# Batch 0's sequence transform as cosine and sine sums, its butterfly in pieces, two more hidden transforms moved ahead of the MLP, powers loaded from ScalarE's queue

## What is computed

```python
# 1. attention with a decaying state, per block of positions
intra = (q @ k.T * D) @ v;  inter = (q * lam_pow) @ kv_state
kv_state = lam_block * kv_state + (k * rev_pow).T @ v
# 2. mixing by a Fourier transform, then an MLP
u = x + real(fft(fft(x, axis=1), axis=2))
un = (u - mean(u)) / sqrt(var(u) + 1e-6)
x = u + relu(un @ w_ch1) @ w_ch2            # 512 -> 2048 -> 512
# 3. a gated unit
gate = sigmoid(causal convolution of x with 5 taps)
out = (gate * (x @ w_val)) @ w_out
```

## Time and profile before

| what | value |
|---|---|
| median of 3 runs | 458.44 us (457.67 to 460.20) |
| the profiled execution's own time | 459.72 us |
| its span, first to last instruction | 457.9 us |
| mean granted TensorE clock | 0.988 |
| TensorE busy | 438.7 us, 96% |
| VectorE busy | 268.2 us, 59% |
| ScalarE busy | 151.9 us, 33% |
| GpSimd busy | 147.0 us, 32% |

### The profile page before, as it was taken

How to read it: one execution, slowest core, us unless ns; L and a number is a source line. 1 busy time by engine, 2 the same in 40 slices (tenths; PEclk the granted TensorE clock), 3 DMA queues, 4 the chain that set the end, 5 groups by cost and what they waited for, 6 DMA issues and landing times.

```text
span 457.9 us, 7070 instructions
## 1 busy us (share of the span) xinstructions
PE 438.7 (96%) x2892; PEld 420.1 (92%) x2892; DVE 268.2 (59%) x419; ACT 151.9 (33%) x284; POOL 147.0 (32%) x99
## 2 busy tenths in 40 slices
PE   6799859999999999999999999999999999999997
PEld 5688749989999999999999999999999999889985
DVE  1657993566835974643533424966565557999220
ACT  1154343065322141111524217344125134525312
POOL 1432536235523222332376422332422450600000
PEclk9899979999999999999999999999999999999999
DMA  6977810050220220202022022022022020001112
GB/s 209 320 219 269 289 67 2 1 183 20 73 94 0 93 77 16 92 1 94 1 93 92 1 92 94 0 93 92 1 92 93 0 93 2 0 1 70 69 47 92
DMA packets 14032, 37.05 MB, mean 81 GB/s; under 512 B 1576, under 2 KB 3120, under 8 KB 14000
## 3 DMA queue, kind: packets, MB, share of 16 engines
q1 hardware_dynamic: 14000, 36.60, 23.8%
HBM read 33.44 MB, written 3.15 MB: 80 GB/s over the span
## 4 chain that ended last, share of the span: by engine, by line
PE 87%; DVE 7%; DMA 3%; ACT 1%; issue 1%; SPq 1%; DVEq 0%
PE ps L550 10%; PE ps L552 9%; PE ps L573 9%; PE ps L572 9%; PE ps L571 9%; PE ps L551 9%; PE ps L489 3%; PE ps L657 2%; PE ps L656 2%; PE ps L655 2%; PE ps L433 2%; PE ps L408 2%; PE ps L634 2%; PE ps L635 2%; PE ps L636 2%; PE ps L444 2%
## 5 line engine op out<-in xcount | busy, mean ns | idle before, releaser
L741 ACT ACTIVATE hh<-ps 128x384 fp32r<-128x384 f32 x64 | 31.5, 492 | 173.1 <-PE ps L552 173.1
L1017 DVE SCALAR_TENSOR_TENSOR hl<-ps,hh 128x384 fp32r<-128x384 f32 x64 | 35.3, 556 | 83.3 <-ACT hh L741 83.3
L550 PE MATMUL ps<-cen_h,w1h_a 128*128 128x384 f32 x128 | 44.1, 344 | 0.5 <-DVE hl L1017 0.5
L550 PE MATMUL ps<-cen_h,w1h_b 128*128 128x384 f32 x128 | 44.2, 345 | 0.0
L552 PE MATMUL ps<-cen_h,w1l_b 128*128 128x384 f32 x128 | 43.1, 337 | 0.0
L552 PE MATMUL ps<-cen_h,w1l_a 128*128 128x384 f32 x128 | 43.1, 337 | 0.0
L573 PE MATMUL ps<-hh,w2l_b 128*128 128x384 f32 x128 | 43.1, 337 | 0.0
L572 PE MATMUL ps<-hl,w2h_b 128*128 128x384 f32 x128 | 43.1, 337 | 0.0
L571 PE MATMUL ps<-hh,w2h_b 128*128 128x384 f32 x128 | 43.1, 337 | 0.0
L551 PE MATMUL ps<-cen_l,w1h_a 128*128 128x384 f32 x128 | 43.1, 337 | 0.0
L551 PE MATMUL ps<-cen_l,w1h_b 128*128 128x384 f32 x128 | 43.0, 336 | 0.0
(11 more groups left out here) (179 smaller groups left out, 1045.5 us busy)
## 6 DMA issues: line engine op xcount, KB each, us to landing
raw_a<-in_mlp SPq DMA_DIRECT2D x16, 512.0 KB, 4.8
raw_b<-in_mlp SPq DMA_DIRECT2D x16, 512.0 KB, 4.4
chunks<-in_qkv SPq DMA_DIRECT2D x12, 512.0 KB, 5.5
chunks<-in_qkv SPq DMA_DIRECT2D x22, 256.0 KB, 4.9
out<-out_sb SPq DMA_DIRECT2D x12, 256.0 KB, 2.0
raw_a<-in_val SPq DMA_DIRECT2D x2, 512.0 KB, 4.5
raw_b<-in_out SPq DMA_DIRECT2D x2, 512.0 KB, 4.6
seq_c<-const_seq SPq DMA_DIRECT2D x1, 768.0 KB, 5.8
```

The lines of the kernel that those rows point to most:

```text
L550: mm(bank, wh_, xh, start=r == 0, stop=False)
L741: nc.scalar.activation(hh[:, slot, j], ps[j][:, 0:TB], ACT.Relu).then_inc(s_hh, 1)
L1017: stt(hl[:, slot, j], ps[j][:, 0:TB], 0.0, hh[:, slot, j].bitcast(F32), ALU.max, ALU.subtract).then_inc(s_hl, 1)
```

## The change

Batch 0 now uses `seq_pair` and `add_pair` too; `seq_tile`, `add_u` and the table part `seq_up` (512 KB) go. The butterfly's operations are the same, but stand at other places: two of the four of `two_pairs` at n = 6, the other two and pair 2 at n = 7, the last six at n = 8. Hidden transforms 6 and 7 move from behind `mean(0)` into chunks 9 and 10, 8 and 9 move behind `mean(0)`, 10 and 11 stay in the MLP; their `radix4` and `spectrum_copy` move along. Tile 2 and 3 of the sequence transform stand behind `from_chunk(10)`. The five instructions on the powers (a write, and three loads behind a wait for it) go from SyncE to the head of ScalarE's queue.

```diff
-            sp.wait_ge(s_pow, 2 + 7)
-            sp.dma_start(rv_dram, rv).then_inc(s_rv, 16)
             load(1, 0, 2, s_tin)
-            sp.wait_ge(s_rv, 16)
-            sp.dma_start(decay[:, :, :], ...
-            for par in range(2):
-                sp.dma_start(qpow[par * Dh:(par + 1) * Dh], ...
             load(1, 2, 3, s_kin)
...
# TensorE
-                elif n <= NC:
+                elif n < NC + 3:
                     pe.wait_ge(s_ye, YE * n)
                 else:
                     pe.wait_ge(s_ye, YE * (n - 1))
-                if n == NC + 1:
+                if n == NC + 3:
                     pe.wait_ge(s_st, 2 * kds(N - 1))
-                if n == NC + 2:
+                if n == NC + 4:
                     pe.wait_ge(s_cen, 4)
...
-                if n == N - 2:
-                    seq_tile(3)
                 from_chunk(n)
                 if n == N - 3:
-                    for a in range(R - 1):
-                        seq_tile(a)
+                    seq_pair(0, 0)
+                    seq_pair(0, 1)
+                    hid_transform(NC)
+                if n == N - 2:
+                    seq_pair(0, 2)
+                    hid_transform(NC + 1)
+                    seq_pair(0, 3)
             mean(0)
-            hid_transform(NC)
-            hid_transform(NC + 1)
+            hid_transform(NC + 2)
+            hid_transform(NC + 3)
...
-        HID_AT = {0: (8,), 1: (9, 10), 2: (11,)}
-        RADIX_AT = {0: (9, 10), 1: (11,)}
+        HID_AT = {0: (10,), 1: (11,)}
+        RADIX_AT = {0: (11,)}
...
# ScalarE
+            act.wait_ge(s_pow, 2 + 7)
+            act.dma_start(rv_dram, rv).then_inc(s_rv, 16)
+            act.wait_ge(s_rv, 16)
+            act.dma_start(decay[:, :, :], ...
+            for par in range(2):
+                act.dma_start(qpow[par * Dh:(par + 1) * Dh], ...
...
                 if n == 9:
                     split_group(0, 0)
                     split_group(0, 1)
+                    spectrum_copy(NC)
+                if n == 10:
+                    spectrum_copy(NC + 1)
             cen_hi(0, 0)
             cen_hi(0, 1)
-            spectrum_copy(NC)
-            spectrum_copy(NC + 1)
+            spectrum_copy(NC + 2)
+            spectrum_copy(NC + 3)
...
# VectorE
-            def two_pairs(b):
+            def two_even(b):
                 y, at = yy[:, b], R6 * b
-                dve.wait_ge(s_r6, at + 3)
+                dve.wait_ge(s_r6, at + 4)
                 tt(y[:, 0], sd[:, 0], sd[:, 1], ALU.add).then_inc(s_r6, 1)
-                dve.wait_ge(s_r6, at + 4)
                 stt(y[:, 1], sd[:, 1], -0.5, sd[:, 0], ALU.mult, ALU.add).then_inc(s_r6, 1)
+
+            def two_odd(b):
+                y = yy[:, b]
                 tt(y[:, 3], sd[:, 3], sd[:, 4], ALU.subtract).then_inc(s_r6, 1)
                 stt(y[:, 4], sd[:, 4], 0.5, sd[:, 3], ALU.mult, ALU.add).then_inc(s_r6, 1)
...
                 if n == NC:
                     chunk_pair(0, 1)
-                    two_pairs(0)
+                    two_even(0)
                 if n == NC + 1:
+                    two_odd(0)
+                    chunk_pair(0, 2)
+                if n == NC + 2:
                     third_pair(0)
-                if n in (8, 9):
-                    radix4(n - 2)
                 if n == N - 3:
-                    for a in range(R - 1):
-                        add_u(a)
-            add_u(3)
+                    radix4(NC)
+                    add_pair(0, 0)
+                    add_pair(0, 1)
+                if n == N - 2:
+                    radix4(NC + 1)
+                    add_pair(0, 2)
+                    radix4(NC + 2)
+                    add_pair(0, 3)
             hidden_sum(0, 3, nc.vector, dve)
+            radix4(NC + 3)
             for hf in range(2):
                 centre(0, hf)
                 cen_lo(0, hf)
             hidden_lo(steps[0])
-            radix4(NC + 2)
+            radix4(NC + 4)
```

More of the change, by code:

```diff
@@ L47, in fourier_constants @@
     parts = []
-    for g in range(G):
+    for g in range(G // 2 + 1):
         th = 2 * np.pi * ((p * (G * np.arange(P)[None, :] + g)) % S) / S
-        c, s, k = np.cos(th), np.sin(th), kappa if g < G // 2 else -kappa
-        parts += [c, s] if g % 3 == 0 else [c, k * s, s, -k * c]
+        c, s = np.cos(th), np.sin(th)
+        parts += [c, s] if g % 3 == 0 else [c, kappa * s, s, -kappa * c]
     seq_tab = np.concatenate(parts, 1).astype(np.float32)
@@ L105, in program @@
         w2l_a = sb("w2l_a", [P, 2, R, P], F32R)
[L107 to L111, removed]
+        hh = sb("hh", [P, 2, 2, TB], F32R)
         hl = sb("hl", [P, 2, 2, TB], F32R)
@@ L191, in program @@
         s_out = [sem(f"s_out{i}") for i in range(2)]
-        HID_AT = {0: (8,), 1: (9, 10), 2: (11,)}
-        RADIX_AT = {0: (9, 10), 1: (11,)}
+        HID_AT = {0: (10,), 1: (11,)}
+        RADIX_AT = {0: (11,)}
         SCORE, COS, SIN, OUT, KV, SPEC = (0, 1), 2, 3, (4, 7), 5, 6
-        SEQ_AT = [P * (2 * ((g + 2) // 3) + 4 * (g - (g + 2) // 3)) for g in range(NC)]
+        SEQ_AT = [P * (2 * ((g + 2) // 3) + 4 * (g - (g + 2) // 3)) for g in range(R)]
         def seq_part(g, i, n=P):
             at = SEQ_AT[g] + i * P
-            return seq_c[:, at:at + n] if g < 4 else seq_up[:, at - LOW_TAB:at - LOW_TAB + n]
-        R4, YE, R6 = 4, 5, 16
+            return seq_c[:, at:at + n]
+        R4, YE, R6, UA = 4, 5, 16, 8
         def spec_bank(n):
-            if n == NC + 1:
+            if n == NC + 3:
                 return ps[KV]
-            return ps[SPEC if n <= NC else (COS, SIN)[n % 2]]
+            return ps[SPEC if n < NC + 3 else (COS, SIN)[n % 2]]
         def added_u(b, a, bank=1):
-            return 2 * a + bank + 1 if b == 0 else 2 * R + 8 * a + 4 * (bank + 1)
+            return UA * (b * R + a) + UA // 2 * (bank + 1)
         TAPS = 2 * (K - 1)
@@ L470, in rows_of, with seq_pair @@
                 return (4, 5) if g in (1, 5) else (1, 2)
-            def seq_tile(a):
+            def seq_pair(b, a):
                 if a == 0:
-                    pe.wait_ge(s_r6, R6)
-                    pe.wait_ge(s_seq, 32)
-                if a == 2:
[L478 to L500, removed]
+                    pe.wait_ge(s_r6, R6 * (b + 1))
+                    if b == 0:
+                        pe.wait_ge(s_seq, 16)
+                    else:
+                        pe.wait_ge(s_ye, YE * N)
+                        pe.wait_ge(s_ve, 2)
+                if a == 2:
+                    pe.wait_ge(s_rev, 4 * (b + 1))
                 for im, bank in ((0, ps[COS]), (1, ps[SIN])):
                     if a:
-                        pe.wait_ge(s_u, added_u(1, a - 1, im))
+                        pe.wait_ge(s_u, added_u(b, a - 1, im))
                     for i, g in enumerate((1, 2)):
@@ L609, in mlp_step @@
                 if 6 <= st.m < 6 + R:
-                    seq_pair(st.m - 6)
+                    seq_pair(1, st.m - 6)
                 if st.m == 10:
@@ L945, in third_pair, with add_pair @@
                 stt(y[:, 4], sd[:, 5], -0.5, y[:, 4], ALU.mult, ALU.add).then_inc(s_r6, 1)
[L948 to L959, removed]
+            def add_pair(b, a):
+                if b and a == 0:
                     dve.wait_ge(s_pv, N)
                     nc.vector.memset(u_pad[1][:, :, 0:PAD], 0.0).then_inc(s_pad, 1)
-                ug = u[1][:, a].rearrange("p (c g) -> p g c", g=NC)
-                xg = xT[:, 1, a].rearrange("p (c g) -> p g c", g=NC)
+                ug = u[b][:, a].rearrange("p (c g) -> p g c", g=NC)
+                xg = xT[:, b, a].rearrange("p (c g) -> p g c", g=NC)
                 to = [lambda v: v[:, 1:3], lambda v: v[:, 0:4:3, 0:P // 2],
```

44 lines of the change are left out of this document (21 added, 23 removed).

## The result

The changed kernel takes 466.51 us, the median of 4 runs (465.32 to 466.97), against 459.12 us (457.67 to 460.20, 4 runs) for the kernel before. The ratio is 1.0159, with a 95% interval of 1.0122 to 1.0196: 7.4 us slower. The forecast was 2.5 us slower, with 464.0 as the upper end. The direction was right, the forecast size was a third of what came. The profiled execution has a span of 464.5 us against 457.9.

What follows compares the result with a forecast made beforehand. TensorE bounded most of the old kernel; VectorE would pace the changed sequence transform. Mean +5.4, clock +0.5, MLP -3.4, start 0 gave +2.5 us on 458.44: 460.9, said as 461.0, range 455.0 to 464.0.

Steps and rivals of the forecast that it cites:

- TensorE's work and the MLP: Sequence transform loses 7.6 us of matmul, yet VectorE sets its pace; two hidden transforms leaving the MLP gain 3.4 us.
- Step 1, the butterfly: VectorE's butterfly, now behind chunk 9's masks and folds, ends at 63.7 us instead of 61.24.
- Step 2, mirror and state ahead of the fold: VectorE's fold of chunk 9 waits for ScalarE's mirror and decay_state; VectorE has nothing to do from 64.9 to 68.0.
- Step 3, two turns behind GpSimd: radix4(6)'s third and fourth operations each wait for a 2.35 us GpSimd weight subtraction: 1.1 + 4.7 us, ending at 74.7.
- The rival with no turn or one turn: radix4(6) escapes GpSimd's subtractions or meets one: 456.3 us (chance 0.22) or about 458.7 (0.10).
- a lead of 0.1 us: Estimated margin by which GpSimd's weight subtraction starts before radix4(6)'s third operation, for both operations to wait.
- Step 4: From tile 0's additions to the mean: slow clock costs 1.9 us, radix4(8) waits 1.75 us; mean 5.4 us later.
- the 0.5 us added for the clock behind it: Hidden transforms 8 and 9 slowed by a lower clock after a 3 us gap before the mean; bounds 0 and 1.5.
- The start: Moved powers and earlier chunk loads at the kernel's start: taken as 0, with ends -1.6 and +2.5 us.
- the second rival: Powers' loads lose turns to chunks; decay used 4 us later, second scores onward 2.5 us later: 463.5 us, chance 0.10.
- the prediction's rule of one instruction each, in turn: VectorE and GpSimd both working on SBUF alternate single instructions; the second waits until the other has finished.

## Why the prediction was right and wrong

- **TensorE's work and the MLP**: right. The products became fewer, the mean came later all the same, and 3.3 us were given back behind it (forecast 3.4). The wait of 0.55 us in MLP step 1 is gone.
- **Step 1, the butterfly**: the end was forecast at 63.7 on the old scale; 69.10 - 5.5 = 63.6.
- **Step 2, mirror and state ahead of the fold**: right. The fold ended at 68.9 on the old scale, as worked out. The runs with the state ahead, or the additions ahead, show it to be one of the two causes in the middle.
- **Step 3, two turns behind GpSimd**: right, 4.3 us of records against 4.7. The rival with no turn or one turn didn't come. The forecast hung on a lead of 0.1 us, but every one of the traces with this order, five of them, shows both turns.
- **Step 4**: the mean was forecast 5.4 us late from this stretch and came 4.4 us late. Two parts were wrong in opposite senses. Tile 1's banks lost 2.6 us to the slow clock, not 1.9, and the hidden transform behind them 0.5 more. And radix4(8) did not wait for GpSimd's hidden sum: it ran at full speed and GpSimd waited, 2.68 us instead of 1.82 (below). So no gap of 3 us opened before the mean, only 1.38 us, and the 0.5 us added for the clock behind it weren't spent.
- **The start: the step that failed.** The term was taken as 0, with +2.5 as its end. (Between 11.58 and 18.70 lie 7.12 us, not 7.15; nothing hangs on that.) It measured +5.5. The mechanism stood in the text as the second rival, with 0.10, and its price was worked out too low in two ways. I let the write land up to 1.5 us earlier because it was no longer behind chunk 0 in one queue; it landed 2.3 us later, because chunks 1 and 2 had moved from behind it to beside it. And I let `decay` come at most 4 us later; its 4.5 us became 8.5, and the two delays add up, since the one transfer waits for the other. That made 6.3 us, of which the vanished wait for chunk 2 gave 1.5 back and the meeting of `radix4` and `decay_keys` took 0.8. A sum of the bytes would have bounded it. SyncE had issued 4.1 MB by 7.8 us (chunks 0 to 2, the hidden table, chunk 3's queries and keys), and by 9.4 us some 2.2 MB had flowed. The rest and the 0.8 MB of the powers' tables are 2.7 MB; at about 350 GB/s they take 7.7 us, as an estimate, and `decay` took 8.4 us. With the start at its true size my sum would have been 5.4 + 0.5 - 3.4 + 5.5 = 8.0, against 7.4 measured.

The forecast of the middle was good to 1 us and its order of events came as written. But of the 7.4 us it explains 1.4, where 2.5 was forecast; the rest is the start's. So that the kernel came out clearly slower was luck in the main: the larger part came from a term that was put at 0.

## What to carry to other kernels

A transfer that all wait for belongs ahead, in the same queue, of those that can come later; moved to another queue it wasn't ahead of them any more but beside them, and took 8.4 us instead of 4.4. Ask of every transfer that is moved what was behind it and is now beside it, and where a load waits for a write, count the price once for each. And when an engine is idle, look at what its next instruction waits for and what is queued behind that one: here moving one call on ScalarE ahead of another was worth 9 us, more than 7.6 us of matmuls taken away.

## What the runs showed of the hardware that was not expected

The turns between VectorE and GpSimd aren't always one instruction each. In the changed kernel radix4(8) and GpSimd's hidden sum (VectorE, then GpSimd):

```profile
97.22 0.44 DVE L891 TENSOR_TENSOR esum<-xT 128x256 f32<-128x256 f32 x1
97.55 0.44 DVE L894 TENSOR_TENSOR zin<-xT 128x256 f32<-128x256 f32 x1
97.89 0.31 DVE L896 TENSOR_TENSOR zin<-esum 128x128 f32<-128x128 f32 x1
98.09 0.31 DVE L897 TENSOR_TENSOR zin<-esum 128x128 f32<-128x128 f32 x1
```

```profile
97.41 2.68 POOL L298 TENSOR_TENSOR out_sb<-out_sb,u_pad 128x768 f32<-128x768 f32 x1 [6.79 <-DVE u_pad L953]
```

GpSimd was released 0.2 us after VectorE's first operation had begun and took 0.86 us more than its 1.82. Worked back from its end (100.09 - 1.82 = 98.27) it got its turn only when VectorE's fourth operation was nearly through; that is an inference, since the record doesn't part waiting from working. So the prediction's rule of one instruction each, in turn, doesn't hold here. At 74.85, released 0.1 us after radix4's second operation had begun, it got its turn after that one. The 2.7 us came in each of the nine traces of the sums form (2.67 to 2.69); why the order differs was not tried. And the write of 8 KB took 3.2, 4.9 or 5.85 us by what was issued beside it.
